# A two-layer network on matrix-memory attention: TensorE takes its steps in pairs

## The reference

```python
B, H, S, D = 4, 8, 768, 40
for t in range(S):                       # matrix-memory attention with input, forget and output gates
    m_new = max(f[t] + m, i[t])
    C = exp(f[t] + m - m_new) * C + exp(i[t] - m_new) * outer(v[t], k[t])
    n = exp(f[t] + m - m_new) * n + exp(i[t] - m_new) * k[t]
    y[t] = sigmoid(o[t]) * (C @ q[t]) / max(abs(n @ q[t]), 1)
x = y.transpose(0, 2, 1, 3).reshape(3072, 320)
h = x @ w_in_1;  x = (max(h, 0) ** 2) @ w_out_1          # 320 -> 2048 -> 320
h = x @ w_in_2;  g = where(h > 0, h, exp(min(h, 0)) - 1) # 320 -> 2048 -> 320
out = g @ w_out_2
```

## Time and profile before

| | before |
|---|---|
| median of 3 runs | 828.01 us (826.4 to 828.03) |
| profiled execution: time / span | 829.19 us / 827.4 us |
| TensorE busy | 818.9 us (99%) |
| VectorE busy | 637.2 us (77%) |
| ScalarE busy | 494.2 us (60%) |
| GpSimd busy | 276.2 us (33%) |
| granted TensorE clock, mean over the span | 0.997 of full speed |

### The profile page before, as it was taken

How to read it: one execution, slowest core, us unless ns; L and a number is a source line. 1 busy time by engine, 2 the same in 40 slices (tenths; PEclk the granted TensorE clock), 3 DMA queues, 4 the chain that set the end, 5 groups by cost and what they waited for, 6 DMA issues and landing times.

```text
span 827.4 us, 14869 instructions
## 1 busy us (share of the span) xinstructions
PE 818.9 (99%) x5251; PEld 813.4 (98%) x5251; DVE 637.2 (77%) x1466; ACT 494.2 (60%) x1096; POOL 276.2 (33%) x289
## 2 busy tenths in 40 slices
PE   9999999999999999999999999999999999999998
PEld 8899999999999999999999999999999999999998
DVE  5799698898897988987965787777768777777642
ACT  4697676776767767767648754444444444444433
POOL 2654232322222423211102353333333333333332
PEclk9999999999999999999999999999999999999999
DMA  8685443443653433436032300000000000000000
GB/s 254 225 241 150 129 117 107 107 120 95 157 152 84 140 107 107 112 102 160 28 105 73 105 2 5 27 4 27 4 27 2 28 3 28 3 27 4 2 25 25
DMA packets 23089, 66.58 MB, mean 80 GB/s; under 512 B 2886, under 2 KB 10214, under 8 KB 20454
## 3 DMA queue, kind: packets, MB, share of 16 engines
q1 hardware_dynamic: 22438, 64.18, 27.3%
q10 hardware_dynamic: 576, 1.44, 0.5%
HBM read 60.87 MB, written 4.03 MB: 78 GB/s over the span
## 4 chain that ended last, share of the span: by engine, by line
PE 95%; DVE 2%; ACT 1%; issue 1%; POOL 0%; ACTq 0%; DVEq 0%
PE hps L1030 43%; PE acc L1044 41%; PE att L954 5%; PE att L916 3%; PE att L945 2%; PE att L933 1%; DVE gate L671 1%; PE acc L982 1%; PE acc L916 0%; PE hps L916 0%; POOL q L372 0%; DVE win L762 0%; PE att L959 0%; DVE win L764 0%; ACT wts L515 0%
## 5 line engine op out<-in xcount | busy, mean ns | idle before, releaser
L1030 PE MATMUL hps<-xth,win 128*128 128x384 f32 x1280 | 351.1, 339 | 0.1
L1044 PE MATMUL acc<-wout,ghi 128*128 128x320 f32 x1536 | 345.5, 311 | 0.0
L1030 PE MATMUL hps<-xtl,win 128*128 128x384 f32 x768 | 259.8, 338 | 0.0
L1044 PEld LDWEIGHTS acc<-wout,ghi 128*128 128x128 f32 x1536 | 259.8, 188 | 0.0
L1044 PE MATMUL acc<-wout,glo 128*128 128x320 f32 x768 | 237.7, 310 | 0.0
L1030 PEld LDWEIGHTS hps<-xth,win 128*128 128x128 f32 x1280 | 229.9, 189 | 0.5 <-DVE xtl L734 0.3
L477 POOL TENSOR_TENSOR glo<-hact,ghi 128x384 fp32r<-128x384 f32 x128 | 130.2, 1017 | 215.4 <-ACT ghi L646 215.4
L1030 PEld LDWEIGHTS hps<-xtl,win 128*128 128x128 f32 x768 | 144.8, 189 | 0.0
L1044 PEld LDWEIGHTS acc<-wout,glo 128*128 128x128 f32 x768 | 144.3, 188 | 0.0
L641 ACT ACTIVATE hact<-hact 128x384 f32<-128x384 f32 x128 | 67.4, 526 | 121.4 <-DVE hact L884 121.4
L851 DVE TENSOR_TENSOR glo<-hact,ghi 128x384 fp32r<-128x384 f32 x128 | 76.8, 601 | 59.5 <-ACT hact L603 58.7
(11 more groups left out here) (146 smaller groups left out, 749.5 us busy)
## 6 DMA issues: line engine op xcount, KB each, us to landing
raw<-in_qk SPq DMA_DIRECT2D x20, 960.0 KB, 7.1
wts<-m_rows SPq DMA_DIRECT2D x24, 512.0 KB, 8.8
kvo<-in_kvo SPq DMA_DIRECT2D x21, 484.0 KB, 7.9
x<-in_w_all SPq DMA_DIRECT2D x12, 352.0 KB, 6.2
wts<-in_w_all SPq DMA_DIRECT2D x12, 352.0 KB, 3.0
q_of_three<-in_q_trios SPq DMA_DIRECT2D x20, 180.0 KB, 3.2
out_x<-hsum SPq DMA_DIRECT2D x16, 160.0 KB, 1.8
x<-in_w_all ACTq DMA_DIRECT2D x4, 352.0 KB, 6.1
```

Source lines behind the costliest of these rows:

```text
L1030: last = nc.tensor.matmul(hps[t % 2][:, 0:NT], win[:, j, w, :], x[:, kk, :], start=(i == 0), stop=(i == len(parts) - 1))
L1044: last = nc.tensor.matmul(acc[u][:, 0:DM], g[t % GR][:, cols], wout[:, j, w, :], start=(j == 0 and i == 0), stop=(j == NF - 1 and i == 2))
```

## The change

```diff
-X2_HI_STEPS = (5, 10, 14)
-X2_LO_STEPS = (5, 10, 15)
-X2_TURNS = (0, 1, 2, 3, 4, 6, 7, 8, 9, 11, 12, 13)
+X2_HI_STEPS = (5, 9, 13)
+X2_LO_STEPS = (6, 10, 14)
+X2_TURNS = tuple(range(12))
...
-    return NF * (g // T - 1) + 5 * (g % T) - 1
+    return max(NF - 1 + 5 * (g - 2 * T), NF * (g // T - 1) + 5 * (g % T) - 3)
...
-                        if j == LAG - 1 and block > 0:
+                        if j == 1 and block > 0:
                             empty_acc(block - 1)
...
-                        if j == LAG - 1:
-                            empty_acc(block - 1)
                         act.wait_ge(s["g_ready"], t + 1)
                         act.wait_ge(s["g_used"], T * (t - GR + 1))
                         nc.scalar.activation(ghi[t % GR][:], gfull[t % 2], ACT.Copy).then_inc(s["ghi_ready"], 1)
+                        if j == 1:
+                            empty_acc(block - 1)
...
-            for block in range(2 * BLOCKS):
-                for j in range(NF):
-                    t = NF * block + j
-                    if j == 0 and block > 0:
-                        second_product(t - LAG)
-                    first_product(t)
...
-                    if t >= LAG and j > 0:
-                        second_product(t - LAG)
...
-            for t in range(2 * BLOCKS * NF - LAG, 2 * BLOCKS * NF):
+            for t in range(NF):
+                first_product(t)
+                attention(t)
+                if t >= LAG:
+                    second_product(t - LAG)
+                g = transposed_at(t)
+                if g is not None:
+                    x1_transposed(g)
+            second_product(NF - LAG)
+            for t in range(NF, 2 * BLOCKS * NF, 2):
+                first_product(t)
+                first_product(t + 1)
+                attention(t)
+                attention(t + 1)
+                second_product(t - 2)
+                second_product(t - 1)
+            for t in range(2 * BLOCKS * NF - 2, 2 * BLOCKS * NF):
                 second_product(t)
```

More of the change, by code:

```diff
@@ L1049, in second_product @@
                     last.then_inc(s["g_used"], T)
-            for block in range(2 * BLOCKS):
-                for j in range(NF):
-                    t = NF * block + j
-                    if j == 0 and block > 0:
-                        second_product(t - LAG)
-                    first_product(t)
[L1057 to L1072, removed]
-                    if t >= LAG and j > 0:
-                        second_product(t - LAG)
-                    g = transposed_at(t)
-                    if g is not None and g < 2 * T:
-                        x1_transposed(g)
@@ L1078, in _, with attention @@
-            for t in range(2 * BLOCKS * NF - LAG, 2 * BLOCKS * NF):
+            def attention(t):
+                block, j = divmod(t, NF)
+                if t in FIRST_STATES:
+                    state_added(FIRST_STATES[t])
+                g = tile_at(t, 0)
+                if g is not None:
+                    scores(g)
+                g = tile_at(t, 2)
+                if g is not None:
+                    if g > T:
+                        state_added(g)
+                    from_state(g)
+                g = tile_at(t, 3)
+                if g is not None:
+                    within(g)
+                if block == BLOCKS - 1 and j in X2_STEPS:
+                    w = X2_STEPS.index(j)
+                    x2_transposed(w, w)
```

## The result

The changed kernel took 834.07 us (median of 4 runs, 833.47 to 834.66) against 827.88 us (826.4 to 828.03, 4 runs): ratio 1.0073, interval 1.0057 to 1.0089. Run again beside the experiments it was 833.09 us against 828.24 us, ratio 1.0059, interval 1.0044 to 1.0073. It is slower by 5 to 6 us, where 830.2 was predicted and the range ended at 833.0; both measured medians lie above that.

A forecast was written before the change was run, and what follows sets the result against it. TensorE, busy for all of layer 1's 330 us, was taken as the bound. A stream shorter by 2.8 us plus 5.0 us of waits gave +2.2 on 828.0, so 830.2 us; range 825.8 to 833.0, 8 in 10.

The forecast's parts named there:

- The side, slower: Whole kernel: slower than before by over 0.2%, given a chance of 0.50; 830.2 us was the main case.
- The three gaps: Layer 1, six-step gaps behind tiles 14, 17, 20: TensorE waits 1.3, 1.3 and 1.9 us.
- the copy met GpSimd's first half: Gaps of layer 1: VectorE's copy in finish meets q's first half by 0.28 us, taking about 1.05 instead of 0.20.
- Layer 2: Blocks of 43.45 us, 0.15 less each, 2.2 us over 15 blocks; no wait of TensorE, none on L889.
- the list of places in layer 1 where a wait can appear: Layer 1: followed each tile's results to the next scores, from_state and F(t0+8), giving waits of 5.0 us in all.
- a wait in the five-step stretch: Layer 1, tiles 7 to 14: TensorE waiting there was named as a sign that the prediction was wrong.
- a tile with an even start ... saves one switch: Layer 1, tiles 7, 9, 11, 13, 16, 19, 22: from_state and within share a pair, saving 7 x 0.09 = 0.6 us.
- +0.09 for second products: TensorE: a second product behind within takes 1.40 instead of 1.31 us, read as the price of switching back.
- The whole gain of the stream: TensorE's own work without waits: 2.2 us from pairs plus 0.6 from saved switches, 2.8 us in all.
- Tiles 20 and 23: Layer 1, even starts with state_added ahead of from_state: from_state waits 0.25 us each, 0.5 in all.
- four and three: Old order behind a gap: the chain was said to meet four first and three second products before the scores.
- the 1.2 us: Profiled execution of before, 829.19 us, against the median of the runs, which lies 1.2 us below it.

The follow-up runs named there:

- layer 2 alone: Kernel before with first and second products paired only in layer 2, its transposes and emptying moved, layer 1 as before: 826.77 us, ratio 0.9978 to before.

## Why the prediction was right and where it failed

- **The side, slower, and its cause were right.** The three gaps were forecast at 1.3, 1.3 and 1.9 us and took 1.4, 1.4 and 2.0 (counted from TensorE's starts against those of undisturbed pairs): the copy met GpSimd's first half by 0.28 us and ended 0.05 behind that half. Moving GpSimd's part took 4.2 us of the steady difference back, which shows the cause.
- **Layer 2 right.** Blocks of 43.47, no wait on L889; shown by layer 2 alone.
- **The step that failed is the list of places in layer 1 where a wait can appear.** It followed tile g's results to `scores`, `from_state` and the relu behind `x_hi`, and left out the user that `first_product` itself names, `xt_ready` at j = 0. Tile 8 starts 7 steps ahead of F(32), and its `x_lo` came 1.3 us late. Moving S(30) ahead took this away. The prediction named a wait in the five-step stretch as a sign that it was wrong, and this is one.
- **A term of the sum was mis-sized: "a tile with an even start ... saves one switch", 0.6 us.** It saves nothing: the switch from `from_state` to `within` costs the 0.08 us that the other one did (2.98 against 2.90). The row behind it, +0.09 for second products, was read as a price of second products and is one of any such change. The whole gain of the stream was 2.1 us, not 2.8.
- **Small sizes.** Tiles 20 and 23 waited 0.36 each instead of 0.25. With 1.3 + 0.6 + 0.3 for the gaps + 0.2 + 0.1 of rounding this is the 2.5 us between the 2.2 forecast and the 4.7 found. (In the old order three first products and three second ones lay between `within` and the scores behind a gap, not four and three as the prediction says; no term of its sum uses this.)
- **From the profile to the median.** The prediction goes by way of the profiled execution, but the 1.2 us cancels: it is before's median, 828.0, plus the sum of 2.2. With the 4.7 us found it would have been 832.7, inside the range and within 0.4 us of the second measurement, 833.09. The first measurement, 834.07, has 1.4 us more, and that part has no cause shown. The bounds had little room for the start of an execution, which varies by 3 us here.

## What to carry to other kernels

When work is regrouped on the engine that bounds the kernel, its own stream may change by hundredths of a microsecond per step (0.02 us per pair here), while the hand-overs to slower chains are re-timed by whole instructions. List the users of each result by the waits in the code, those at loop boundaries too, and compare for each the work that now lies between. Where GpSimd and VectorE work side by side, count a slack below the length of one GpSimd instruction (1.29 us here) as none, until a trace shows that the two don't block each other. A table of starting steps and the step at which a shared queue empties a buffer are one decision: the new starts with the old emptying cost 10.8 us here, of which 1.6 were a lower clock behind the first wait.

## What the runs showed of the hardware that I had not expected

- Changing from one kind of matmul to another on TensorE costs some 0.02 to 0.03 us with 384 and 320 columns: over the pairs of layer 2 a first product takes 1.415 us behind a second one and 1.387 behind another first one, a second product 1.312 behind a first one and 1.320 behind another second one. It costs 0.06 to 0.09 us out of the attention pieces, between two attention pieces as well (2.98 for both against 1.20 + 1.70).
- VectorE obtains its turn between two GpSimd instructions that follow each other at once: a copy that takes 0.20 us alone ended 0.05 us behind the first of two halves that the records show end to end. Not every VectorE instruction is blocked: one that reads `att`, which lies in PSUM, the memory that TensorE writes its products to, kept its 0.49 us beside GpSimd's q part in the kernel before, whose halves run from 181.19 to 183.72:

```profile
182.10 0.49 DVE L726 TENSOR_TENSOR x<-att,rden 128x320 f32<-128x320 f32 x1
```

- TensorE's granted clock fell to 0.50 behind the first wait of 2.2 to 2.4 us in two kernels, with 1.6 and 1.7 us of slower matmuls, and didn't fall behind the later waits of the same length.
- Steady stretches repeat to 0.1 us between executions (733.5 and 733.5 us for the changed kernel, and 43.47 us for each plain block of layer 2), but the start of F(16) varies by 3 us.
